# A delta-rule chunk loop in front of two MoE layers: queries-times-state products spread into two other stages, and a new order of weight loads and operand splits

## The reference, cut to what matters

```python
# attention: B=4, H=8, S=768, D=48
for t in range(S):
    y[:, :, t] = einsum('bhd,bhde->bhe', q[:, :, t], state)
    v_old = einsum('bhde,bhd->bhe', state, k_n[:, :, t])      # k_n: k divided by its norm
    state = state + beta_t * einsum('bhd,bhe->bhde', k_n[:, :, t], v_t - v_old)
# moe: x is y as [3072, 384], d_ff = 1536
x = (x @ w_a) * (x @ w_b) @ w_out
# moe2: 8 experts, one for each token
e_idx = argmax(x @ w_gate + modality_bias[modality_id])
out[mask] = gate_w[mask] * (relu(x[mask] @ w1[e]) @ w2[e])
```

## Time and profile before

| | us |
|---|---|
| three runs | 1034.84, 1031.45, 1037.15 (median 1034.84) |
| profiled execution | 1034.84, its span 1033.0 |
| TensorE busy | 911.3 (88%) |
| VectorE, ScalarE, GpSimd busy | 494.9, 274.0, 314.0 |
| mean granted clock of TensorE | 0.967 |

### The profile page before, as it was taken

How to read it: one execution, slowest core, us unless ns; L and a number is a source line. 1 busy time by engine, 2 the same in 40 slices (tenths; PEclk the granted TensorE clock), 3 DMA queues, 4 the chain that set the end, 5 groups by cost and what they waited for, 6 DMA issues and landing times.

```text
span 1033.0 us, 26546 instructions
## 1 busy us (share of the span) xinstructions
PE 911.3 (88%) x10756; PEld 797.4 (77%) x10757; DVE 494.9 (48%) x1027; ACT 274.0 (27%) x505; POOL 314.0 (30%) x567
## 2 busy tenths in 40 slices
PE   1846799999889898899999999999847999999995
PEld 1835687878768787787888887889746999999995
DVE  4754776566546655476546654343472222222221
ACT  2103223222213132322323222323302232223221
POOL 0212133343333233343334343333401222222221
PEclk9999799999989899999999999999958999999999
DMA  7868357866485667755775676443547411181110
GB/s 205 313 160 248 93 188 205 241 212 205 138 198 169 203 198 203 227 179 188 203 193 170 187 214 185 167 154 126 182 154 270 141 46 38 38 289 42 36 44 24
DMA packets 149796, 172.44 MB, mean 167 GB/s; under 512 B 108975, under 2 KB 115505, under 8 KB 148160
## 3 DMA queue, kind: packets, MB, share of 16 engines
q0 software_dynamic: 31232, 115.44, 32.9%
q1 hardware_dynamic: 118464, 55.54, 21.2%
HBM read 101.74 MB, written 69.40 MB: 166 GB/s over the span
## 4 chain that ended last, share of the span: by engine, by line
PE 65%; DMA 13%; DVE 11%; issue 5%; ACT 3%; POOL 2%; SPq 0%; DVEq 0%; POOLq 0%; ACTq 0%
PE pab L564 11%; PE pab L566 10%; PE pab L565 10%; DMA work<-we_in 7%; PE pto L564 3%; PE pto L566 3%; PE pto L565 3%; PE px L499 2%; DVE work L1047 2%; DVE work L1051 2%; ACT work L799 2%; PE px L564 2%; DVE work L1093 2%; PE px L566 2%; PE px L565 2%
## 5 line engine op out<-in xcount | busy, mean ns | idle before, releaser
L1459 POOL DMA_DIRECT2D expert_split_scratch<-work x128 | 69.6, 543 | 380.0 <-DVE work L1093 379.7
L564 PE MATMUL pab<-wbuf,x_hi 128*128 128x512 f32 x432 | 181.2, 419 | 1.2 <-DVE x_lo L1103 1.2
L566 PE MATMUL pab<-wbuf,x_lo 128*128 128x512 f32 x432 | 172.3, 399 | 1.4 <-issue 1.4
L565 PE MATMUL pab<-wbuf,x_hi 128*128 128x512 f32 x432 | 172.7, 400 | 0.1
L1093 DVE TENSOR_TENSOR work<-work 128x384 fp32r<-128x384 f32 x128 | 76.2, 596 | 129.6 <-ACT work L799 129.4
L564 PE MATMUL pto<-wbuf,g_hi 128*128 128x392 f32 x288 | 104.6, 363 | 26.7 <-DVE g_lo L1116 13.9
L799 ACT ACTIVATE work<-work 128x384 fp32r<-128x384 f32 x128 | 66.3, 522 | 130.0 <-DMA work<-we_in 130.0
L566 PE MATMUL pto<-wbuf,g_lo 128*128 128x392 f32 x288 | 99.5, 346 | 0.0
L565 PE MATMUL pto<-wbuf,g_hi 128*128 128x392 f32 x288 | 99.4, 345 | 0.0
L564 PEld LDWEIGHTS pab<-wbuf,x_hi 128*128 128x128 f32 x432 | 82.6, 191 | 21.3 <-issue 1.8
L566 PEld LDWEIGHTS pab<-wbuf,x_lo 128*128 128x128 f32 x432 | 82.8, 192 | 19.7
(11 more groups left out here) (176 smaller groups left out, 1627.7 us busy)
## 6 DMA issues: line engine op xcount, KB each, us to landing
expert_split_scratch<-work POOLq DMA_DIRECT2D x256, 192.0 KB, 3.3
work<-we_in POOLq DMA_DIRECT2D x128, 192.0 KB, 4.0
work<-a_in POOLq DMA_DIRECT2D x12, 1792.0 KB, 8.1
wbuf<-expert_split_scratch SPq DMA_DIRECT2D x24, 768.0 KB, 5.8
work<-wm_in POOLq DMA_DIRECT2D x18, 384.0 KB, 6.0
work<-a_in SPq DMA_DIRECT2D x12, 512.0 KB, 4.6
inverse_in_scratch<-work SPq DMA_DIRECT2D x12, 512.0 KB, 7.0
work<-a_in SPq DMA_DIRECT2D x6, 768.0 KB, 7.0
```

Source lines behind the costliest of these rows:

```text
L564: pe.matmul(o, a_hi, w_hi, start=first, stop=False)
L565: pe.matmul(o, a_hi, w_lo, start=False, stop=False)
L566: return pe.matmul(o, a_lo, w_hi, start=False, stop=last)
L1459: pool.dma_start(ws_hi[e, c], s_hi[j % 2].bitcast(F32)).then_inc(s_hs[j % 2], 16)
```

## The change

It does five things.

1. qs_products(c) as a stage is gone. Its calls for p = 0 stand in across(c), those for p = 1 in second_block(c), two after the four calls of each head u; across waits for kqm, and the semaphore qs goes.
2. In odd slots ScalarE copies a_copy(t,2) before hi_piece 2, and hi_piece 3, 4 and 5 all stand ahead of g_split(t,2) and x_split(n). VectorE does lo_piece 3 ahead of norm_root and at_form, lo_piece 4 ahead of g_split(t,2), and the NEXT part of the inverse behind x_split.
3. The dense weights go through six buffers at first (the ring's four, a_u and a_w), then the ring of four. GpSimd issues ten loads before the first triangle instead of four, and four loads behind v_scale(0).
4. kk_products(2) and (3) stand ahead of the gate products.
5. Every load_out_t of GpSimd (parts 5 and 6) waits for the split that frees a_u or a_w, and stands behind load_row(0); load_dense 15 stands ahead of triangle(1).

```diff
         def staged(i):
-            return raw_ring[i % 4]
+            return flat((a_u, a_w)[i - 4]) if i in (4, 5) else raw_ring[i if i < 4 else (i - 6) % 4]
+
+        def staged_count(i):
+            return 16 if i < 6 else 16 * ((i - 6) // 4 + 2)
...
-            def qs_products(c):
-                pe.wait_ge(S["kqm"], c + 1)
-                for u in range(U):
-                    e = slice(u * HD, (u + 1) * HD)
-                    for p in range(2):
-                        for h in HALF:
-                            f, o = feature_rows(p, h), output_rows(p, h)
-                            mm = pe.matmul(px[o:o + CH, p, e], queries_of(p, u, f), a_s[f:f + HD, p, e],
-                                           start=(u == 0), stop=False)
-                mm.then_inc(S["qs"], 1)
+            def qs_products(p, u):
+                e = slice(u * HD, (u + 1) * HD)
+                for h in HALF:
+                    f, o = feature_rows(p, h), output_rows(p, h)
+                    mm = pe.matmul(px[o:o + CH, p, e], queries_of(p, u, f), a_s[f:f + HD, p, e],
+                                   start=(u == 0), stop=False)
+                return mm
...
             def across(c):
                 pe.wait_ge(S["ucp"], c + 1)
                 pe.wait_ge(S["tw"], 32 * (c + 1))
+                pe.wait_ge(S["kqm"], c + 1)
...
                                            start=True, stop=True)
+                    if c >= 1:
+                        qs_products(0, u)
                 mm.then_inc(S["vmm"], 1)
...
             def second_block(c):
...
+                    if c >= 1:
+                        mm = qs_products(1, u)
                 mm.then_inc(S["umm"], 1)
...
             def y_and_s(c):
                 pe.wait_ge(S["w"], c + 1)
-                pe.wait_ge(S["kqm"], c + 1)
-                if c >= 1:
-                    pe.wait_ge(S["qs"], c)
...
                 second_block(c)
-                qs_products(c)
                 b_products(t, 1)
...
-            kk_products(0)
-            kk_products(1)
+            for c in range(AHEAD):
+                kk_products(c)
             pe.wait_ge(S["small"], 48)
             for i in range(PARTS):
                 gate_products(i)
-            kk_products(2)
-            kk_products(3)
...
             def hi_dense(i):
-                act.wait_ge(s_rd[i % 4], 16 * (i // 4 + 1))
+                act.wait_ge(s_rd[i if i < 6 else (i - 6) % 4], staged_count(i))
...
                 hi_piece(n, 1)
+                a_copy(t, 2)
                 hi_piece(n, 2)
-                a_copy(t, 2)
                 g_split(t, 1)
-                hi_piece(n, 3)
...
                 if norm < GROUPS:
                     sqrt(norm)
+                hi_piece(n, 3)
                 hi_piece(n, 4)
+                hi_piece(n, 5)
                 g_split(t, 2)
                 if n < STEPS:
                     x_split(n)
-                hi_piece(n, 5)
...
-            for i in range(4):
+            for i in range(6):
                 hi_dense(i)
             square(1)
-            for i in range(4, 8):
+            for i in range(6, 10):
                 hi_dense(i)
...
                 g_form(t, 2)
+                lo_piece(n, 3)
                 if norm < GROUPS:
                     norm_root(norm)
                 if n // 2 + AHEAD < PAIRS:
                     at_form(n // 2 + AHEAD)
-                lo_piece(n, 3)
+                lo_piece(n, 4)
                 g_split(t, 2)
                 if n < STEPS:
                     x_split(n)
-                lo_piece(n, 4)
-                if n < STEPS:
                     sub_part(n, NEXT)
                 lo_piece(n, 5)
...
             def load_dense(i):
-                if i >= 4:
-                    pool.wait_ge(S["lo"], i - 3)
-                pool.dma_start(staged(i), wm_in[:, dense_columns(i)]).then_inc(s_rd[i % 4], 16)
+                if i >= 6:
+                    pool.wait_ge(S["lo"], i - 5 if i < 10 else i - 3)
+                place = i if i < 6 else (i - 6) % 4
+                pool.dma_start(staged(i), wm_in[:, dense_columns(i)]).then_inc(s_rd[place], 16)
 
             def load_out_t(i):
+                pool.wait_ge(S["lo"], i)
...
             pool.wait_ge(S["kk"], 2)
-            for i in range(4):
+            for i in range(10):
                 load_dense(i)
             triangle(0)
+            load_row(0)
             load_out_t(5)
             load_out_t(6)
-            load_row(0)
-            for i in range(4, 8):
-                load_dense(i)
             v_scale(0)
-            for i in range(8, 12):
+            for i in range(10, 14):
                 load_dense(i)
             load_row(1)
-            for i in range(12, 15):
+            for i in range(14, 16):
                 load_dense(i)
             triangle(1)
-            for i in range(15, ND):
+            for i in range(16, ND):
                 load_dense(i)
```

More of the change, by code:

```diff
@@ L230, in build @@
         hh0 hh1 tw row v2 rq rsub u1 ucp vmm radd umm w ysmm sadd kqmm kqm ycp
-        xtr xh xl am bm acp gm gtr gh gl outmm y2sb rd0 rd1 rd2 rd3 qs
+        xtr xh xl am bm acp gm gtr gh gl outmm y2sb rd0 rd1 rd2 rd3 rd4 rd5
         lsb ost small wt0 wt1 wt2 wt3 wt4 wt5 wt6 wgm wgh wgl rch rexp rex rpe rtab grow tabmm raw0 raw1 hi lo wdone hs0 hs1 ls0 ls1 rord
@@ L237, in build @@
         s_hh = [S["hh0"], S["hh1"]]
-        s_rd = [S[f"rd{i}"] for i in range(4)]
+        s_rd = [S[f"rd{i}"] for i in range(6)]
         s_wt = [S[f"wt{i}"] for i in range(PARTS)]
@@ L925, in _ @@
             x_split(0)
-            for i in range(8, 12):
-                hi_dense(i)
+            hi_dense(10)
+            hi_dense(11)
             odd_slot(1)
@@ L1241, in _ @@
             x_split(0)
-            for i in range(8, 12):
-                lo_dense(i)
+            lo_dense(10)
+            lo_dense(11)
             odd_slot(1)
```

## The result

| | before | changed |
|---|---|---|
| median of the runs beside each other, us | 1035.99 (1031.45 to 1038.33) | 1119.83 (1111.82 to 1129.5) |
| ratio, 95% interval | | 1.0789 (1.0708 to 1.0872) |
| span of the profiled execution, us | 1033.0 | 1119.3 |
| mean granted clock of TensorE | 0.967 | 0.937 |

A forecast was written before the change was run, and what follows sets the result against it. It took TensorE, busy 88% of 1033.0 us, as the bound, so longer TensorE work is paid in full. 45 - 3 + 15 + 2 = +59 on 1034.84 gave 1094 us, range 1038 to 1122.

The forecast's parts named there:

- The largest term: TensorE's size changes from moving qs into across and second_block: +45 us, bounds 38 to 51.
- Counting changes of size: In across and second_block: 29 more size changes a chunk pair at 0.14 us, 4.1 us x 11 = 45 us.
- The clock: Rival, chance 0.07: broken even-slot stretches or new odd-slot waits bring TensorE's lower clock, +20 to +35 us, 1114 to 1129.
- The odd slots: New ScalarE and VectorE order: TensorE waits for g_lo behind piece 5, +15 us, bounds -5 and +25.
- The waits that the longer stretches were to cover: Small waits in front of second_block are covered by the longer stretches: 0.3 us a pair, -3 us.
- The start: Before the first out_products: later gate products cost +5 us, fewer loads behind triangle(1) give back 3; +2, bounds -4 and +8.
- The overlap rival: Across and qs calls of both sizes run together in different tiles, the 2.00 us run vanishes: -22 us, 1030; chance 0.17.
- part 1: The qs calls moved into across and second_block, 11 chunk pairs: +45 us for size changes, -3 for covered waits.
- the other parts: The new odd-slot order, +15 us, and the start, +2 us: 17 us.

The follow-up runs named there:

- e4: As e1, but the qs calls stand behind every second head, in rounds twice as long: 1056.43 us, ratio 1.0209 to the kernel before.
- e6: As e1, but each qs call is cut into two of 32x32, leaving out query features 32 to 47: 1062.64 us, ratio 1.0202 to the kernel before.
- e1: The kernel before with only the qs calls moved inside across and second_block: 1087.96 us, ratio 1.0513.
- e2: The kernel before with only the new order of ScalarE and VectorE in odd slots: 1067.84 us, ratio 1.0331.
- e5: The kernel before with h run backwards for p = 1 in qs, so that tiles alternate: 1033.86 us, ratio 1.0003.
- parts 1, 2 and 3: Each alone on the kernel before: qs calls in across and second_block, 1.0513; odd-slot order, 1.0331; points 3 to 5 of the change, 1.0023.
- e9: The kernel before with qs in its own run, each call cut into two of 32 output rows: 1055.01 us, ratio 1.0191.

## Why the prediction was right, and where it was short

The largest term was right by its mechanism. That the time as a whole fell inside the range was in part luck: two terms came out larger than forecast, and the upper end of 1122 had been set by a rival given a chance of 0.07.

- **Counting changes of size (34 instead of 5 in a chunk pair).** Right. 3.8 us a stretch were forecast, 3.72 measured; 4.1 us a pair, 3.8 measured; 45 us in all, 42 measured. e4 gives 0.13 us a change and e6 takes the size away. The two rows it rested on, one size overlapping by 0.10 us and another starting 0.06 us after, carry the whole term.
- **The clock.** This is the step that fell short. The forecast's sum had no term for it; it stood as a rival with chance 0.07 (+20 to +35), and came. About 27 us of the 86 are half clock. e1 shows more of it with the stretches and with less idle time than before, e2 with the new waits. I had argued from the run of qs at full clock, which is 2.0 us long; the new stretches are 3.7 us long and e4's, at 2.67 us, hardly show it.
- **The odd slots.** The mechanism was right: g_hi behind a piece that has not landed. The term was mis-sized: +15 forecast with bounds of -5 and +25, +36 measured by the medians of e2; in its profiled execution it is 33.6 us, of which 12 are clock and 21 idle time. For the five slots without norm it was near: 14.4 us together in the changed kernel (2.94 in slot 21), 13.5 forecast. The four early slots were forecast at +1.5 together, because the later wait at first_block was to pay for the new one. They wait 4.4 to 6.8 us each (slot 5: 6.24, not 4 to 5), 22.7 together, and had held 14.9 before (1.62 and 4.62 for g_lo, 0.65, 3.87 and 4.12 at first_block): +7.8. So the waits were 6 to 7 us more than forecast, and the clock, 12 us, had been left out.
- **The waits that the longer stretches were to cover (-3 us).** TensorE's idle time in e1 is 8.6 us below before, a little more than that.
- **The start.** Forecast +2, measured +3 within an interval that includes 0. Its parts were larger: the key products waited until 47.89 us, where the forecast had load 3 landed by 43, so SP's store was 10 us late, outside the bounds of +1 and +9, and as much was given back.
- **The overlap rival.** Its argument, tiles in alternation overlap, falls with e5: the same two tiles in strict alternation take 2.00 us as before. Its limit was also added up wrongly: at 0.05 us a change part 1 would gain 0.5 x 11 = 6 us against 17 us of the other parts, so the kernel would still be 11 us slower; it is faster only below 0.016 us.
- Added singly, parts 1, 2 and 3 are +5.1%, +3.3% and +0.2%, 8.7%; together they are 7.9%, so they overlap little.

## What to carry to other kernels

Filling gaps on TensorE with small products of another tile size did not pay: each change cost 0.13 us, more than the two records it let in (0.06). With the size of their neighbours the stretches were shorter (e6), but no run here turned that into time. Before moving an operation ahead of others on an in-order engine, ask what it waits for; one split ahead of two others cost 3% because its DMA came 2 to 6 us later. And stretches with many changes of size can be followed by the lower clock although no idle time is shown, so price them twice.

## What the runs showed of the hardware

- Half clock without any idle time: 3.4 us at 0.50 behind a stretch of 3.7 us with 17 changes of size (e1; a piece in or behind nine of 22 stretches, ten of 22 in the changed kernel), in one of 22 when the stretch is 2.67 us with 9 changes (e4).
- The pace of small products goes by the tile. 64 records of 48x64 spread over four tiles take 0.93 us (L473), over two 2.00 us (L499), in either order of the two (e5); with 32 columns over four tiles 128 records take 1.49 us (e9).
- TensorE stopped for up to 3.93 us inside a run of small records, waiting for nothing shown (e9). All 43 such stops of over 0.5 us in the fourteen traces end 2.2 to 3.3 us after an instruction transfer of 16 KB has started; the kernel before has three, the longest 1.25 us, e9 eight.
